# A fused recurrent attention and two feed-forward layers on one core: in each slot, the first layer's elementwise steps are issued ahead of the attention's instead of between or behind them

## The reference, cut to what matters

```
# 1: gated linear attention, 4 x 8 heads, 768 steps, head size 48
f = sigmoid(f_logit)
state = f[t] * state + outer(k[t], v[t]);  y[t] = q[t] @ state
# 2: first layer, x = y as (3072 tokens, 384)
h = x @ w_in                                  # 384 -> 2048
g = where(h >= 1, h, where(h <= -1, 0, (h + 1)**2 / 4))
x = g @ w_out                                 # 2048 -> 384
# 3: second layer
x = (silu(x @ w_gate) * (x @ w_val)) @ w_out  # 384 -> 1536 -> 384
```

## Time and profile before

| | |
|---|---|
| median of three runs | 1079.31 us |
| the profiled execution | 1078.47 us, of which its span is 1076.7 us |
| TensorE matmul busy | 1015.5 us, 94% of the span |
| VectorE, ScalarE, GpSimd busy | 547.0, 445.2, 450.8 us |
| granted clock of TensorE, mean | 0.979 of full speed |

### The profile page before, as it was taken

The page is one execution under the profiler, slowest core; times in us unless marked ns, Lnnn a source line. Parts: engine busy times, 40 slices in busy tenths (PEclk is TensorE's granted clock), DMA queues, the critical chain, the costliest instruction groups (busy, mean ns, idle before and its releaser), DMA issues.

```text
span 1076.7 us, 19206 instructions
## 1 busy us (share of the span) xinstructions
PE 1015.5 (94%) x7816; PEld 828.8 (77%) x7816; DVE 547.0 (51%) x745; ACT 445.2 (41%) x808; POOL 450.8 (42%) x368
## 2 busy tenths in 40 slices
PE   2477899999999999999999999999999999999997
PEld 2465677778778777877788888888888888888886
DVE  7965965884686488568736532223222222222221
ACT  3439538544753855375336532122222222222221
POOL 3956962763564476447327422121221212212121
PEclk9569999999999999999999999999999999999999
DMA  9423005003300600220043110010010010000000
GB/s 357 158 72 145 1 2 216 31 2 124 122 1 2 216 30 2 82 107 2 2 177 131 45 39 22 1 59 1 1 59 1 1 59 1 30 1 1 30 1 29
DMA packets 17367, 63.52 MB, mean 59 GB/s; under 512 B 1920, under 2 KB 2176, under 8 KB 16512
## 3 DMA queue, kind: packets, MB, share of 16 engines
q1 hardware_dynamic: 17280, 62.30, 15.8%
HBM read 52.85 MB, written 9.44 MB: 58 GB/s over the span
## 4 chain that ended last, share of the span: by engine, by line
PE 83%; issue 5%; DVE 5%; ACT 3%; POOL 3%; DMA 1%; SPq 0%; POOLq 0%; ACTq 0%; DVEq 0%
PE acc L445 10%; PE acc L447 10%; PE acc L446 10%; PE bank L473 7%; PE bank L471 7%; PE bank L472 7%; PE hid L431 6%; PE bank L344 5%; PE hid L432 5%; PE hid L433 5%; DVE scores L748 3%; PE hid L473 2%; PE hid L472 2%; PE hid L471 2%; PE bank L376 2%
## 5 line engine op out<-in xcount | busy, mean ns | idle before, releaser
L939 POOL TENSOR_TENSOR g_lo<-prod,g_hi 128x512 fp32r<-128x512 f32 x72 | 93.1, 1293 | 347.4 <-ACT g_hi L650 347.4
L932 POOL TENSOR_TENSOR g_lo<-act_tmp,g_hi 128x512 fp32r<-128x512 f32 x96 | 140.5, 1463 | 188.8 <-ACT g_hi L611 188.8
L837 DVE TENSOR_TENSOR sig<-sig,bank 128x512 f32<-128x512 f32 x72 | 49.6, 688 | 275.9 <-ACT sig L644 275.9
L748 DVE COPY_PREDICATED scores<-mask,bank 64x512 f32<-64x512 int32 x144 | 134.2, 932 | 28.4 <-PE bank L344 26.6
L650 ACT CAST g_hi<-prod 128x512 fp32r<-128x512 f32 x72 | 44.9, 624 | 247.6 <-PE acc L447 247.6
L892 POOL TENSOR_TENSOR keys<-keys,gates 128x512 f32<-128x512 f32 x82 | 110.2, 1343 | 44.1 <-PE bank L344 32.7
L611 ACT CAST g_hi<-act_tmp 128x512 fp32r<-128x512 f32 x96 | 59.6, 621 | 164.1 <-DVE act_tmp L825 164.1
L344 PEld LDWEIGHTS bank<-right_q,keys 128*64 128x64 f32 x2304 | 81.0, 150 | 58.8 <-issue 54.6
L344 PE MATMUL bank<-right_q,keys 128*64 128x64 f32 x2304 | 91.0, 238 | 36.0 <-ACT right_q L546 28.1
L445 PE MATMUL acc<-g_hi,wout_hi 128*128 128x512 f32 x288 | 117.0, 406 | 8.0 <-POOL g_lo L932 8.0
L431 PE MATMUL hid<-x_hi,win_hi 128*128 128x512 f32 x288 | 119.0, 413 | 4.0 <-DVE act_tmp L825 4.0
(11 more groups left out here) (80 smaller groups left out, 1851.6 us busy)
## 6 DMA issues: line engine op xcount, KB each, us to landing
gates<-in_f_dram SPq DMA_DIRECT2D x12, 512.0 KB, 5.3
queries<-in_q_dram SPq DMA_DIRECT2D x12, 512.0 KB, 5.4
keys<-in_k_dram SPq DMA_DIRECT2D x12, 512.0 KB, 4.7
values<-in_v_tok_dram SPq DMA_DIRECT2D x6, 1024.0 KB, 8.8
q_tok<-in_q_tok_dram SPq DMA_DIRECT2D x12, 384.0 KB, 8.6
k_tok<-in_k_tok_dram SPq DMA_DIRECT2D x12, 384.0 KB, 9.0
x_dram<-x_out SPq DMA_DIRECT2D x6, 768.0 KB, 3.9
x_raw<-x_dram SPq DMA_DIRECT2D x6, 768.0 KB, 5.5
```

Of the source, the lines that this page charges most:

```text
L748: last = dve.copy_predicated(o, level_mask(li, half), t[rows(half), :].rearrange("p (x b r) -> p x b r", x=BP, r=m))
L932: pool.tensor_tensor(g_lo[:, c % RING, :], act_tmp[:, 2 + c % 2, :], g_hi[:, c % RING, :].bitcast(F32), ALU.subtract).then_inc(g_lo_done, 1)
```

## The change

Chunk c's slot, on each engine, before and after (att is the attention of a half slot):

- VectorE: att(2c), activate(c-1), clamp(c), att(2c+1) becomes activate(c-1), clamp(c), att(2c), att(2c+1).
- ScalarE: square(c-1), att(2c), split_g1(c-1), att(2c+1) becomes split_g1(c-1), att(2c), square(c), att(2c+1).
- GpSimd: att(2c), split_g1(c-1), att(2c+1) becomes split_g1(c-1), att(2c), att(2c+1).

TensorE's and the DMA queue's instructions stay. No instruction is added or removed.

```diff
 # scalar
-                    square(*((m, c - 1) if c else (m - 1, FC1 - 1)))
+                    split_g1(*((m, c - 1) if c else (m - 1, FC1 - 1)))
                 for a, place in turns(m, 2 * c):
                     attention(a, place)
-                if m > 0 or c > 0:
-                    split_g1(*((m, c - 1) if c else (m - 1, FC1 - 1)))
+                square(m, c)
                 for a, place in turns(m, 2 * c + 1):
                     attention(a, place)
...
-                    square(UNITS - 1, FC1 - 1)
                     split_g1(UNITS - 1, FC1 - 1)
 # vector
-                for a, place in turns(m, 2 * c):
-                    attention(a, place)
                 if m > 0 or c > 0:
                     activate(*((m, c - 1) if c else (m - 1, FC1 - 1)))
                 clamp(m, c)
+                for a, place in turns(m, 2 * c):
+                    attention(a, place)
 # gpsimd
+                if m > 0 or c > 0:
+                    split_g1(*((m, c - 1) if c else (m - 1, FC1 - 1)))
                 for a, place in turns(m, 2 * c):
                     attention(a, place)
-                if m > 0 or c > 0:
-                    split_g1(*((m, c - 1) if c else (m - 1, FC1 - 1)))
```

## The result

The changed kernel takes 1086.78 us (median of 4 runs, 1085.89 to 1087.15) against 1079.12 us before: a ratio of 1.0070, 95% interval 1.0053 to 1.0088. It is slower by 7.7 us; 4.0 to 4.4 were forecast. Its profiled execution has a span of 1085.4 us, 8.7 more than before.

A forecast was written before the change was run, and what follows sets the result against it. TensorE, busy 1015.5 of 1076.7 us, was taken as the bound, so only its idle time counts. Terms 3.9 + 0.9 - 0.5 + 0.1 made +4.4 us, given as 1083.3 us, range 1079.5 to 1087.

The forecast's parts named there:

- Two of the signs that the prediction names: No TensorE wait in dense slots of units 1 to 4; long VectorE idle before unit 0 clamps, delaying TensorE, would refute.
- Term 1, the unit ends: Ends of units 1 to 3: additions behind the clamp and a late query copy idle TensorE, +1.3 each, +3.9 us.
- The end of unit 0: End of unit 0: square ahead of key copies and the same late query copy, +0.9 us (0 to 1.5).
- Term 2, unit 0: Unit 0's dense slots: the 1.76 us low-part wait goes, a 0.6 us key wait comes; -0.5 us with the start.
- against that stands the start: Start of unit 0: one more square, 0.52 us, delays GpSimd, and VectorE must once wait for a hidden product.
- Term 3: Unit 5's weight splits: a ring of 4.4 us against a slot of 4.08 us, +0.1 us (0 to 1).
- Covered at nothing: the dense slots: Dense slots of units 1 to 4: 1.5 us to spare in the even half slot, 0.5 in the odd; no cost.
- The rival of the waiting dense slots: Odd half's take-overs outlast their mean, so levels wait 14 steps in 4 or 5 units: 1096 us; chance 0.12.

The follow-up runs named there:

- slot-13 run: Changed kernel with slot 13 reordered: VectorE's additions to the state between maximum and clamp, ScalarE's square behind the state copy in units 1 to 3; 1081.30 us.
- run with VectorE alone: Only VectorE's part of the change kept, ScalarE and GpSimd as in the kernel before; 1086.88 us, ratio 1.0073 against the kernel before.

## Why the prediction was right in kind and short in size

- **Bound and way.** TensorE's idle time was the measure, the low part's waits fell (8.0 to 3.7 us), and new waits outweighed it. 1086.78 us lies just inside the range, whose upper end was 1087.0; the point was 3.5 us low. That it lies inside is partly luck: the forecast's terms make 4.4 us, the traces 8.7, and nearly half of those come from a place that was put at nothing. Two of the signs that the prediction names went against it: TensorE did wait in the dense slots, and VectorE did stand idle for 2.59 us before a clamp in unit 0.
- **Term 1, the unit ends: right in mechanism and size.** Forecast +1.3 each, measured +1.2. Idle time of ScalarE before square and copy, no change of the projection's start against the start of slot 13 worth naming, the query copy late, TensorE waiting 1.19 us for it: each is in the trace. Less the 2.00 us by which slot 13 starts later, the copy of the state begins at 268.18 (268.2 was forecast), the cast of chunk 14 at 277.98 (278.05), and the copy of the queries ends at 283.50 (283.45). Against 282.43 that last one makes 1.0 us of wait, where the prediction wrote 1.1. The slot-13 run shows the hold behind the clamp to be worth 2.1 us, the 0.75 that it leaves being the late query copy. The trace also has the gating at 1.44 us, where the earlier trace rows has 1.23 alone: 0.2 of the 0.4 that I allowed for the low part beside it.
- **The end of unit 0** was put at +0.9. The landmarks go from 1.1 at 138 us to 0.9 at the first level, so it cost nothing: the new wait of 1.21 us before the level was paid for by two old waits that went, which I had not subtracted.
- **Term 2, unit 0: the wrong sign.** Forecast -0.5, measured +1.1 at 138 us. The wait of 1.76 us for the low part did go, and one of 0.49 us for scaled keys came, as foretold. What failed is the step "against that stands the start": I let one square and one stall of VectorE stand for it. In fact TensorE, earlier by 2.3 us, ran into one idle time of 4.72 us, came back at half clock and made VectorE wait 2.59 us. With ScalarE's start as before, the term is -0.4 in that run's trace, 1.5 us less than in the changed kernel's.
- **Term 3** is zero: the landmarks do not move behind 530 us.
- **"Covered at nothing: the dense slots": the step that failed, 4.2 us.** The links were the right ones (take-over, scaling, maximum, cast, copy), but the slots and the durations were not.
  - *Half slot 5, 0.6 us a unit.* The prediction reckoned with slots of 6.4 us "at least", with two levels each. The slots before this level hold one level and are 5.4 us long (282.43 to 287.81 before). From the hidden product of slot 1, at 286.68, to the start that the level would have had without its wait, at 296.4, there are 9.7 us. At the prediction's durations the links make 2.04 + 0.69 + 1.86 + 1.05 + 0.69 + 0.6 + 1.3 = 8.2, so 1.5 to spare. But the first levels are taken over in 2.65 us, not twice 0.93, and the scaling beside GpSimd's key scaling takes 1.96, not 1.05: 1.7 us more, and nothing is left. The remaining 0.4 us lie between the engines.
  - *Half slot 13 (the expectations call it 14), 0.3 us, and half slot 17, 0.1.* In slot 5 of unit 2, ahead of the 0.3 us, the take-overs are short, 1.45 us each. But VectorE is busy for 22.6 of the 23 us from 301 to 324, against 20.3 in the same stretch before, and comes to its clamp at 313.58, 1.1 us after the end of the hidden product. That VectorE is idle for 28 of 100 us was no protection, since the idle time lies elsewhere.
  - The rival of the waiting dense slots had the mechanism and too high a price, 11 to 14 us, since I let all 14 steps wait; three of them do.

## What to carry to other kernels

When an instruction is moved ahead on an in-order engine, list what now stands behind each wait that it brings, and work the chain with the durations of the very slots it crosses: means over the whole kernel hid 1.7 us here. An order can be good in one phase and bad in another; here the cast first paid at the unit ends, where ScalarE is full, and cost in the dense slots, where the queries' copy is urgent, and the version with the order of ScalarE and GpSimd chosen by phase, and VectorE's left alone, was 0.7% faster than the old kernel while the uniform change was 0.7% slower.

## What the runs showed of the hardware that was not expected

- TensorE's granted clock fell to 0.50 behind an idle time of 4.72 us in one piece and stayed there until some 5.5 us after the work had begun again. The four other runs with the same order at the start of unit 0 had one piece of 4.75 to 5.55 us, and 0.50 behind it too. In the kernel before and in the run with unit 0's old start, with 1.0 and 2.0 us in two pieces, it stayed at 1.00; so it did behind one piece of 2.75 us, in the run with the attention ahead of the cast everywhere. But the run with VectorE alone had two pieces of 0.93 and 1.98 us, and its clock was 0.67 from 96 to 98 us and 0.50 from 98 to 100. So neither the number of pieces nor their sum decides it, and what does stays open.
- The scaling of the queries, 128x512 on VectorE with both inputs in SBUF, takes 0.69 us alone and 1.96 us when GpSimd's scaling of the keys starts 0.12 us ahead of it. The Trainium skill (SBUF — State Buffer, "Who interferes with whom") has such a pair lock each other out, whoever starts first. The trace agrees for the one order that it shows, GpSimd first: the keys' scaling ended at 293.75, and the queries' at 294.31, about one bare duration later.
